# Unused products in TensorE's pauses, and the first slots of a fused convolution and two-layer feed-forward kernel reordered

## The reference

```python
w = softmax(weight)                     # 8 heads x 7 taps
out[b, s] = sum_k w[h, k] * x_pad[b, s + k]   # 24 features share a head
```

```python
h = x @ w_in;  g = h * cos(h);                   x = g @ w_out     # layer 1
h = x @ w_in;  g = h * clip(h + 3, 0, 6) / 6;    out = g @ w_out   # layer 2
```

## Time and profile before

| | |
|---|---|
| median of 3 runs | 2235.25 us (2234.97 to 2236.0) |
| the profiled execution, its own time | 2235.39 us |
| its span in the trace | 2233.6 us |
| TensorE (PE) busy | 2224.0 us, 100% of the span |
| VectorE (DVE) busy | 1823.6 us, 82% |
| ScalarE (ACT) busy | 1732.6 us, 78% |
| GpSimd (POOL) busy | 1514.7 us, 68% |
| mean granted TensorE clock | 0.999 |

### The profile page before, as it was taken

How to read it: one execution, slowest core, us unless ns; L and a number is a source line. 1 busy time by engine, 2 the same in 40 slices (tenths; PEclk the granted TensorE clock), 3 DMA queues, 4 the chain that set the end, 5 groups by cost and what they waited for, 6 DMA issues and landing times.

```text
span 2233.6 us, 56658 instructions
## 1 busy us (share of the span) xinstructions
PE 2224.0 (100%) x19491; PEld 2200.1 (98%) x19491; DVE 1823.6 (82%) x2505; ACT 1732.6 (78%) x2841; POOL 1514.7 (68%) x1071
## 2 busy tenths in 40 slices
PE   9999999999999999999999999999999999999999
PEld 6899999999999999999999999999999999999998
DVE  8978888888888888888888888888888888888754
ACT  7888777787777877778877788777787777877775
POOL 7976666666666666766666666666666666666665
PEclk9999999999999999999999999999999999999999
DMA  4200000000000000000000000000000000000001
GB/s 107 58 8 16 15 10 4 14 14 14 14 0 14 14 14 14 0 14 14 14 14 7 7 14 14 14 13 1 14 14 14 14 0 14 14 14 7 4 6 23
DMA packets 208636, 33.27 MB, mean 15 GB/s; under 512 B 203152, under 2 KB 207248, under 8 KB 208592
## 3 DMA queue, kind: packets, MB, share of 16 engines
q1 hardware_dynamic: 205424, 32.27, 8.2%
q10 hardware_dynamic: 3168, 0.39, 0.1%
HBM read 19.92 MB, written 12.58 MB: 15 GB/s over the span
## 4 chain that ended last, share of the span: by engine, by line
PE 98%; DVE 1%; ACT 0%; DMA 0%; SPq 0%; issue 0%; DVEq 0%
PE h_ps L475 47%; PE acc L482 31%; PE acc_tail L489 21%; DVE acc L1002 0%; DMA x_in<-in_x 0%; DVE gate L930 0%; ACT pre L754 0%; DVE pre L919 0%; DVE wtail_hi L1044 0%; ACT pre L744 0%; ACT g_hi L758 0%; SPq L433 0%; ACT in_hi L887 0%; DVE acc L1001 0%; DVE xT L967 0%
## 5 line engine op out<-in xcount | busy, mean ns | idle before, releaser
L1186 POOL TENSOR_TENSOR g_lo<-gate,g_hi 128x512 fp32r<-128x512 f32 x1024 | 1470.5, 1458 | 702.1 <-ACT g_hi L758 701.2
L482 PE MATMUL acc<-g_hi,wout 64*128 64x512 f32 x4096 | 1416.4, 386 | 0.0
L475 PE MATMUL h_ps<-in_hi,win_hi 64*128 64x512 f32 x2048 | 790.7, 387 | 1.7 <-ACT in_hi L887 1.3
L489 PE MATMUL acc_tail<-g_lo,wout 64*128 64x512 f32 x2048 | 791.0, 386 | 0.0
L475 PE MATMUL h_ps<-in_lo,win_hi 64*128 64x512 f32 x2048 | 790.9, 387 | 0.0
L489 PE MATMUL acc_tail<-g_hi,wout 64*128 64x512 f32 x2048 | 790.7, 386 | 0.0
L482 PE MATMUL acc<-g_lo,wout 64*128 64x512 f32 x2048 | 790.4, 386 | 0.0
L475 PE MATMUL h_ps<-in_hi,win_lo 64*128 64x512 f32 x2048 | 790.3, 387 | 0.0
L475 PE MATMUL h_ps<-in_tail,wtail_hi 64*128 64x512 f32 x2048 | 790.0, 387 | 0.3 <-DVE in_tail L1069 0.3
L482 PEld LDWEIGHTS acc<-g_hi,wout 64*128 64x128 f32 x4096 | 753.4, 184 | 2.7 <-issue 0.3
L758 ACT ACTIVATE g_hi<-gate 128x512 fp32r<-128x512 f32 x1024 | 624.1, 631 | 114.1 <-DVE gate L933 55.0
(11 more groups left out here) (121 smaller groups left out, 2371.7 us busy)
## 6 DMA issues: line engine op xcount, KB each, us to landing
out_dram<-o_blk SPq DMA_DIRECT2D x128, 64.0 KB, 1.8
x_in<-in_x SPq DMA_DIRECT2D x126, 64.0 KB, 2.2
blk_tail<-in_x SPq DMA_DIRECT2D x62, 64.0 KB, 2.2
out_dram<-blk_tail SPq DMA_DIRECT2D x62, 64.0 KB, 1.8
stage<-in_moe_w_out SPq DMA_DIRECT2D x7, 384.0 KB, 3.3
stage<-in_moe_w_in SPq DMA_DIRECT2D x3, 512.0 KB, 4.4
stage<-in_moe_w_in SPq DMA_DIRECT2D x6, 256.0 KB, 3.9
pre<-in_moe_w_in SPq DMA_DIRECT2D x2, 256.0 KB, 4.6
```

The source lines that it names most:

```text
L475: return pe.matmul(chunk_of(h_ps, q, half), w, x, start=start, stop=stop)
L482: return pe.matmul(acc[pair][:, :], wout[layer][rows, 2 * q + half, cols], g[rows, :], start=start, stop=stop)
L489: return pe.matmul(acc_tail[pair][:, :], wout[layer][rows, 2 * q + half, P:2 * P], g[rows, :], start=start, stop=stop)
L1186: pool.tensor_tensor(chunk_of(g_lo, q, half), chunk_of(gate, q, half), chunk_of(g_hi, q, half).bitcast(F32), ALU.subtract).then_inc(glo_re ...
```

## The change

- `bridge(n)` issues n pairs of products of the high part of w_in with itself into the bank of h that slot 1 uses; nobody reads them. Five pairs stand between the tail convolutions and slot 0, and one behind the third unit of slot 0.
- The last four upper units of slot 1 are issued by themselves at the end of slot 1, no longer beside slot 2's. Those of slots 0 and 2 stay beside the next slot's.
- TensorE's taps 0 and 1 of tile 1 are issued behind slot 1 and behind slot 2, where they stood at the fifth step of slot 1 and of slot 2.
- ScalarE's high part of slot 0, half 0, is made in slot 1, behind the copies of h of slot 1.
- VectorE casts piece 7 in slot 2 (it was slot 1), and its taps of tile 1 are dealt out differently. GpSimd makes piece 7's low part ahead of slot 3 (it was slot 2).
- The kept columns move from slot 0 to 6 on ScalarE, the low part of tile 1's tail from slot 2 to slot 7 on VectorE.

```diff
+BRIDGE_PAIRS = 5
-        HIGH_BY_DVE = {0: {0: 6, 1: 7, 3: 8, 5: 9}, 1: {0: 10, 1: 11, 2: 12, 4: 13, 7: 14}}
+        HIGH_BY_DVE = {0: {0: 6, 2: 7, 3: 8, 5: 9}, 1: {0: 10, 1: 11, 2: 12, 4: 13, 7: 14}}
-        LOW_IN = {1: 6, 2: 7, 4: 8, 6: 9, 8: 10, 10: 11, 12: 12, 14: 13, 16: 14, 18: 15, 20: 16, 22: 17}
+        LOW_IN = {1: 6, 3: 7, 4: 8, 6: 9, 8: 10, 10: 11, 12: 12, 14: 13, 16: 14, 18: 15, 20: 16, 22: 17}
-        CONV_FIRST = [2, 2, 3, 5, 6, 7, 7, 7, 7]
+        CONV_FIRST = [2, 2, 3, 4, 5, 7, 7, 7, 7]
-        KEEP_1, TWIN_1, TAIL_1, LOW_TAIL_1, HIGH_1, LOW_1 = 0, 1, 2, 2, 5, 6
+        KEEP_1, TWIN_1, TAIL_1, LOW_TAIL_1, HIGH_1, LOW_1 = 6, 1, 2, 7, 5, 6
...
-                if 0 < q <= LAG and i < 4:
+                if q in (1, LAG) and i < 4:
                     first_upper(5 + i, ph, q - 1, ph.base + q - 1)
-                if 0 < q <= SECOND_BY_PE and i == 4:
-                    convolve_second(q - 1)
...
                     if i < 9:
                         first_lower(i, ph, q, ph.base + q)
+                    if q == 0 and i == 2:
+                        bridge(1)
                     if i >= 5:
                         first_upper(i - 5, ph, q, ph.base + q)
+                if q == 1:
+                    for i in range(5, 9):
+                        first_upper(i, ph, q, ph.base + q)
+                if q > 0:
+                    convolve_second(q - 1)
...
+            def bridge(count):
+
+                w = win_hi[L1]
+                for _ in range(count):
+                    for rows, half in ((LOW, 0), (UP, 1)):
+                        pe.matmul(chunk_of(h_ps, 1, half), w[rows, 0:P], w[rows, 0:TOK], start=True, stop=True)
...
             convolve_tails()
+            pe.wait_ge(whi_done, 1)
+            bridge(BRIDGE_PAIRS)
             phase(first_phase())
...
                     before_gate(ph.layer, q, slot)
+                    if ph.setup == 0 and q == 1:
+                        high_half(0, 0, 0)
                     if ph.setup in (0, 1) and slot > 0:
                         high_half((q - 1) % SLOTS, slot - 1, 1)
...
-                    high_part(q, slot, ph.setup != 0 or q >= G_BUFS, 1 if ph.setup in (0, 1) else 2)
+                    if ph.setup != 0 or q > 0:
+                        high_part(q, slot, ph.setup != 0 or q >= G_BUFS, 1 if ph.setup in (0, 1) else 2)
```

## The result

| | before | changed |
|---|---|---|
| median | 2236.05 us (12 runs, 2234.97 to 2236.48) | 2241.70 us (12 runs, 2239.21 to 2243.67) |
| the profiled execution, its own time | 2235.39 us | 2239.49 us |
| its span | 2233.6 us | 2237.8 us |
| slot 8's first unit | 48.75 us | 51.60 us |

The ratio is 1.0026 with a 95% interval of 1.0019 to 1.0034: slower, by 5.65 us between the medians, a quarter of a percent. The forecast was 2239.3, in a range of 2236.0 to 2242.3. The median lies beyond 2239.7, where the prediction let "slower" begin, and that side it had given 0.43 against 0.54 for "same".

What follows compares the result with a forecast made beforehand. TensorE was taken to bound the kernel, with 98% of the time to the end running through it. From 2235.4 us, -1.35 (front), +3.7 (slot 8's pause) and +1.6 (clock) gave 2239.3 us, range 2236.0 to 2242.3.

Steps and rivals of the forecast that it cites:

- The pause of slot 8: TensorE's slot 8 waits for tile 1's low tail behind VectorE's slot 7 gates: 3.9 us pause, +3.7 us with nothing gained ahead.
- Rival (c): At slot 8: the low tail isn't last, its split ends before about 47.3, no pause; 2233.7 us, chance 0.05.
- The clock behind the pause: Behind slot 8's pause TensorE's granted clock falls to half for a stretch: +1.6 us, bounds 0 and 2.8.
- Rival (a): At slot 8: the pause costs no clock, TensorE being at work right around it; 2237.7 us, chance 0.13.
- The bridge: Unused products around slot 0's start fill TensorE's pauses: themselves 0 us, clock held through the 3.4 us stretch, -1.7 us.
- what they bring is the clock: Unused products before and in slot 0 keep the granted clock from falling at 15.5 us: -1.7 us, bounds -1.7 and 0.
- Slot 1 by itself: At slot 1's end its last four upper units lose their partners on TensorE: 4 x 0.226 = +0.9 us.
- The stalls of slots 3 to 7: Gate waits of 0.64 + 0.31 us up to slot 6 go, piece 7's lateness returns 0.55; gain 1.35 us by slot 7.
- The sum: Whole kernel: 2235.4 - 1.35 (front) + 3.7 (slot 8's pause) + 1.6 (clock behind it) = 2239.3 us, +0.18%.

Runs made afterwards that it cites:

- experiment 2: Kernel before with only the low part of tile 1's tail moved from VectorE's slot 2 to slot 7; median 2240.02 us, ratio 1.0025.
- experiment 7: The changed kernel measured and profiled again, unaltered; median 2241.34 us, ratio 1.0030 against the kernel before.
- experiment 1: Changed kernel with the low part of tile 1's tail back in VectorE's slot 2; median 2235.56 us, ratio 1.0004.
- experiment 11: Changed kernel with the low part of tile 1's tail in VectorE's slot 6 instead of 7; median 2236.16 us, ratio 1.0004.
- experiment 8: The kernel before measured and profiled again, unaltered, one round; median 2234.54 us, ratio 1.0000.
- experiment 4: Changed kernel with the low part of tile 1's tail back in slot 2 and no unused products; median 2236.35 us, ratio 1.0008.
- experiment 5: Kernel before with only the unused products added, five pairs behind the tails and one in slot 0; median 2235.21 us, ratio 1.0000.
- experiment 10: Kernel before with only the low part of tile 1's main part in VectorE's slot 5 instead of 6; median 2234.51 us, ratio 0.9997.
- experiment 6: Kernel before with the unused products and the low part of tile 1's main part in VectorE's slot 5; median 2233.56 us, ratio 0.9998.
- experiment 3: Changed kernel with slot 8's pause filled by 16 further pairs of unused products; median 2238.01 us, ratio 1.0017.
- experiment 12: Kernel before plus unused products, low parts of tile 1's main part in VectorE's slot 5 and tail in slot 4; median 2232.70 us, ratio 0.9993.
- experiment 9: Changed kernel with tile 1's low tail back in slot 2 and TensorE's old order of slots 1 to 3; median 2235.85 us, ratio 1.0003.

## Why the prediction was right

**The pause of slot 8: right, in kind and in size.** Forecast: 3.9 us of pause behind the gates of slot 7, 0.69 us of split and 0.06 us to TensorE. Measured: 51.60 - 47.50 = 4.10 us between the time at which slot 8's first unit was due and its start, 3.72 of them with TensorE idle; 0.69 and 0.06. It came out that well as the length is that of a chain that the trace of before already had (7.55 us from a slot's first unit to the end of its gates, 50.82 - 43.20 = 7.62 here). It was the same when the slot began earlier: 4.10 us and 3.72 idle in experiments 2 and 7 too. Experiments 2, 1 and 11 show the cause from three sides: put alone it costs 5.3 us, put back the wait for it is gone, and one slot earlier its split is done as slot 8 is due. Rival (c) would have needed the split before 47.3; it came at 51.54.

**The clock behind the pause: right in kind, short for the median.** Forecast 1.6 us, bounds 0 and 2.8. The first profile had 1.35, the second 2.51, and filling the pause gave back 2.3 to 3.1 us of the medians. Rival (a) fell with that. This is likely the larger part of why the median is at 2241.7 and the first profiled execution at 2239.49, next to the forecast of 2239.3: the forecast took a stretch as long as the one of the earlier trace rows, and in another execution it lasted twice as long. I had named that as a bound. How long it lasts in the executions without a profile isn't shown.

**The bridge: right for the execution forecast from, wrong as a saving.** Its cover held to 0.1 us (slot 0 at 13.32 instead of 13.21), and the clock was 1.00 at 15.5 us. But the 1.7 us were a property of one execution. In the profile of before the clock fell at the front, in the ones of experiments 2 and 8 it held with nearly the same pauses. It held in all nine profiles with the products, but in four of the five without them too, so the profiles don't show that the products hold it. And where full clock comes later (4, 5, 10, 11: the tails end at 13.7 us or later instead of 11.9), the pause between the tails and slot 0 that the bridge was to fill isn't there, and its pairs push slot 0, by 0.6 us at the low-tail unit. The step that failed is "what they bring is the clock": in some executions 1.4 us (12.46 - 11.03), in some nothing, in some a loss.

It also bears on the spread of the kernel before. Every run has its mean granted clock on record, to three digits. A stretch of 3.4 us at 0.5 takes 1.7 / 2234 = 0.0008 off it, so a run at 1.000 had none. Of the 112 runs of the kernel before that the experiments brought, 35 are under 2234 us. 31 lie between 2234 and 2235.1, and 23 of these have 1.000, so it wasn't a fall of the clock that made them slow; experiment 10 has a profile at such a time (2234.51), and there full clock came late. 46 are above, and none of these has 1.000, which fits the fall in the profiled run at 2235.39. That these two are what parts the groups is likely and not shown run by run. With the bridge alone ten of 11 runs have 1.000, against nine of the 30 runs of before in that call, and yet six of the 11 are above 2235.2: there the products seem to hold the clock, and the late start costs what they save.

**Slot 1 by itself: right, +0.9 forecast.** With the clock held, the old order takes 11.03, 10.95, 11.00, 11.03 and 11.02 us from the low-tail unit to the fifth pair of slot 3 (experiments 2, 5, 6, 8, 10), and the new one 11.76, 11.77, 11.73, 11.79 and 11.76 (the changed kernel, 1, 3, 4, 7): +0.75 us. Experiments 12 (old order, 11.20) and 11 (new order, 11.66) lie a little closer together. Experiment 9 was to show it in one run and failed. So that mark came at 26.27, forecast 26.1.

**The stalls of slots 3 to 7: partly.** The stalls at slots 5 and 6 were forecast to go and piece 7 to be late by 0.4 to 1.3 us. Piece 7 was late by 0.41 us, and the next pair by 0.11 more. TensorE wanted it 38 pairs behind the mark, at 34.89, where the forecast counted 37. From the mark to the time at which slot 8 was due it took 47.50 - 26.27 = 21.23 us for 91 pairs that need 20.60, so 0.63 us were lost, forecast 0.55; 0.11 of them I haven't located. Slot 7 started 44.29 - 43.20 = 1.09 us before it did in the profile of before; the forecast had 1.35. That term was a quarter of a microsecond too large. The chain from slot 7's first unit to the end of its gates was 0.19 us longer than in the profile of before (7.62, it was 51.72 - 44.29 = 7.43). With both slot 8 comes at 51.6 and not 51.1. What I had not separated is why these stalls went: experiment 1 has the whole change but the late low tail, and stalls at slots 5, 6 and 8 (34.80, 39.43, 48.96). It was the low tail's leaving slot 2 that relieved VectorE: with that edit alone (experiment 2) no unit of slots 3 to 7 is late. The costly edit also carried the gain, and experiment 12 keeps the gain by moving it to slot 4, not 7. One edit works the other way, and the prediction had it at nothing: with TensorE's taps behind slots 1 and 2, VectorE's first tap of tile 1 waits for the second of them, 1.19 us in the changed kernel and 1.42 in experiment 1, which it doesn't in any profile with the old order. What that wait costs by slot 8 wasn't separated.

**The sum.** -1.09 (slot 7) + 3.94 (slot 8, 51.60 - 47.50, less the 0.16 that it was late before) + 1.35 = 4.2 us between the two profiled executions, forecast -1.35 + 3.7 + 1.6 = 3.95. The three terms were off by +0.26, +0.24 and -0.25, and two of these cancel. That part of the agreement is luck. So is which executions were profiled: the one of before had the fall at the front, and the first one after had the short stretch behind the pause. Between the medians the change costs 5.65 us in one measurement and 6.4 in the other.

## What to carry to other kernels

When a hand-dealt schedule moves a small operation to a later slot, look up what it feeds and in which slot of *the consumer* the wait stands. Slot 7 of VectorE and slot 8 of TensorE look one behind the other in the tables, but TensorE wanted slot 8 at 47.50 us and VectorE's gates of slot 7 ended at 50.82; so a split of 0.69 us behind them held slot 8 for 4.1 us, and the same split one slot earlier next to nothing. Price a pause of TensorE twice, once for its length and once for the clock behind it, and look at more than one profile before you call a slow stretch a fixed cost that filling can save. If moving an operation away relieves a queue, ask which later slot has room and still ends ahead of the need, and count what else is queued in it.

## What the runs showed of the hardware that wasn't expected

The granted clock at the front isn't the same from one execution of one kernel to the next. The kernel before, with TensorE idle for 1.28 and 1.14 us ahead of slot 0 and again before the low-tail unit, fell to 0.50 for 3.4 us once and stayed at 1.00 once. The full clock at the very start comes at different times too: the trace's record of it begins between 4.8 and 6.7 us in ten profiles and between 10.2 and 11.0 in four (4, 5, 10, 11). The first half of the tails took 2.8 to 2.9 us in the former and 4.6 to 5.0 in the latter, and slot 0 starts at 13.70 and 13.77 us in the two of these without the products, instead of 13.02 to 13.21. The Trainium skill ("TensorE: Matmul & The Clock Gate", "What's actually happening") calls the number of slow matmuls at a kernel's start run-variable, and the two groups here agree with it. Behind the same pause of 3.72 us the half-clock stretch was 3.4 us long in two profiles (the changed kernel, experiment 2) and 6.8 us in one (experiment 7).
